# q and k multiplied by the decays channel by channel, and brought to heads through DRAM instead of by transposes

## The reference

```
mag = sqrt(a_re^2 + a_im^2);  a = (a_re, a_im) * min(mag, 0.999) / (mag + 1e-6)
for t in tokens:   S = a[t] * S + k[t] (x) v[t]        # complex S, 48 x 48 per head; k, v real
                   y[t] = q[t] . real(S)
```

## Time and profile before

| | |
|---|---|
| runs | 2439.87 us median of 3 (2435.78 to 2443.03) |
| profiled execution | 2443.79 us, its span 2442.0 us |
| TensorE busy | 2307.7 us, 95% of the span; granted clock 0.985 in the mean |
| VectorE, ScalarE, POOL busy | 1035.7, 763.4, 332.4 us |
| DMA | 106.63 MB in 95411 packets, 44 GB/s |

### The profile page before, as it was taken

One profiled execution on the slowest core, in us unless ns is written; L12 is line 12 of the kernel. 1 busy time (PEld: TensorE's weight loads), 2 busy tenths in 40 slices (PEclk: granted clock), 3 DMA queues, 4 the chain that ended last, 5 costly groups with the idle time before them and its releaser, 6 DMA issues.

```text
span 2442.0 us, 36281 instructions
## 1 busy us (share of the span) xinstructions
PE 2307.7 (95%) x14011; PEld 2150.2 (88%) x14011; DVE 1035.7 (42%) x2073; ACT 763.4 (31%) x1519; POOL 332.4 (14%) x423
## 2 busy tenths in 40 slices
PE   3699999999999899999999999999999999999999
PEld 3699999999999888998999999999999899989998
DVE  7787888888873333222222222222222222222222
ACT  3455555555545411222211222211222221222211
POOL 0000000000001211111111111111211111111100
PEclk8699999999999999999999999999999999999999
DMA  3211111111111400111011111041111110111001
GB/s 103 78 40 35 47 47 47 47 46 47 47 40 45 152 27 27 35 36 35 29 30 29 35 35 35 28 145 31 35 35 36 29 30 29 35 35 35 29 13 26
DMA packets 95411, 106.63 MB, mean 44 GB/s; under 512 B 9448, under 2 KB 89576, under 8 KB 95208
## 3 DMA queue, kind: packets, MB, share of 16 engines
q1 hardware_dynamic: 95208, 103.99, 13.8%
HBM read 89.80 MB, written 14.16 MB: 43 GB/s over the span
## 4 chain that ended last, share of the span: by engine, by line
PE 82%; DVE 8%; ACT 6%; issue 2%; DMA 1%; POOL 0%; SPq 0%; ACTq 0%; DVEq 0%
PE bank L1105 14%; PE bank L1106 14%; PE bank L1107 14%; PE bank L1224 11%; PE bank L1225 11%; PE bank L1226 11%; PE bank L1092 2%; PE bank L1091 2%; PE bank L1096 1%; PE bank L1086 1%; ACT ubuf L564 1%; ACT ubuf L566 1%; ACT ubuf L562 1%; PE bank L1081 1%; DVE an L707 1%
## 5 line engine op out<-in xcount | busy, mean ns | idle before, releaser
L660 ACT ACTIVATE h_h<-bank 128x512 fp32r<-128x512 f32 x384 | 229.8, 598 | 1254.7 <-PE bank L1107 1245.5
L1224 PE MATMUL bank<-w_h,h_h 128*128 128x384 f32 x1536 | 516.4, 336 | 0.0
L1226 PE MATMUL bank<-w_h,h_l 128*128 128x384 f32 x1536 | 516.3, 336 | 0.0
L1225 PE MATMUL bank<-w_l,h_h 128*128 128x384 f32 x1536 | 516.2, 336 | 0.0
L961 DVE SCALAR_TENSOR_TENSOR h_l<-bank,h_h 128x512 fp32r<-128x512 f32 x384 | 265.3, 691 | 530.2 <-ACT h_h L660 529.8
L490 POOL TENSOR_TENSOR w_l<-stage,w_h 128x256 fp32r<-128x256 f32 x384 | 286.2, 747 | 1296.4 <-ACT w_h L642 1296.2
L1105 PE MATMUL bank<-x2h,w_h 128*128 128x512 f32 x1152 | 451.1, 392 | 3.2 <-issue 2.4
L1106 PE MATMUL bank<-x2l,w_h 128*128 128x512 f32 x1152 | 451.1, 392 | 0.0
L1107 PE MATMUL bank<-x2h,w_l 128*128 128x512 f32 x1152 | 448.4, 389 | 0.0
L974 DVE SCALAR_TENSOR_TENSOR acc<-bank,prob,acc 128x384 f32<-128x384 f32 x168 | 103.8, 618 | 578.9 <-PE bank L1226 578.9
L1224 PEld LDWEIGHTS bank<-w_h,h_h 128*128 128x128 f32 x1536 | 288.1, 188 | 1.9
(11 more groups left out here) (134 smaller groups left out, 2771.5 us busy)
## 6 DMA issues: line engine op xcount, KB each, us to landing
stage<-w_ SPq DMA_DIRECT2D x384, 128.0 KB, 2.1
qb<-q_in_ SPq DMA_DIRECT2D x24, 192.0 KB
kb<-k_in_ SPq DMA_DIRECT2D x24, 192.0 KB
vb<-v_in_ SPq DMA_DIRECT2D x24, 192.0 KB
x_hi<-x2h_s SPq DMA_DIRECT2D x36, 128.0 KB, 1.9
x_lo<-x2l_s SPq DMA_DIRECT2D x36, 128.0 KB, 1.8
x2h<-x_hi SPq DMA_DIRECT2D x6, 768.0 KB, 8.7
x2l<-x_lo SPq DMA_DIRECT2D x6, 768.0 KB, 10.2
```

The source lines that it names most:

```text
L660: act.activation(h_h[:, f], hc[f % 3][:], ACT.Relu).then_inc(hh_done, 1)
L1224: pe.matmul(dst, h_h[:, f, t_], w2s[slot][0][:, f], start=f == 0, stop=False)
L1225: pe.matmul(dst, h_h[:, f, t_], w2s[slot][1][:, f], start=False, stop=False)
L1226: mm = pe.matmul(dst, h_l[:, f, t_], w2s[slot][0][:, f], start=False, stop=f == NF2 - 1)
```

## The change

**Products.** q and k themselves are transposed to channels (`q_turn`, `k_turn`, three transposes each), and VectorE multiplies them there: q by both parts of p in one instruction (`by_q`, into `qp`), k first by `rr` (into `pm`) and then by both parts of p (`by_k`, into `kp`). POOL's `pinv` is gone.

**To heads.** SP stores `qp` and `kp` to DRAM as [part, channel, token] and loads them back as `qs` and `ks`, with the 48 channels of a head on partitions 0 to 47 (real) and 48 to 95 (imaginary): two stores and four loads a unit, in pieces of 512 bytes. k with tokens on partitions (`kt`, for the state) comes from `ks` by eight transposes (`k_back`), copied by ScalarE (`k_by_token`).

**Order.** A unit has 9 steps on TensorE. Unit `u` carries the four tiles from `t = 4 * (u - 2) - 1`, and nine tiles follow behind unit 23. On TensorE three `mm_in` and two `mm_out` stand between the turns and `k_back`. The lists of ScalarE and VectorE are written anew. The gate goes to `att[2]`. `araw` and `r_sum` have more room, y a buffer of its own.

```diff
 def to_heads(u):                                   # SP, new
+    if u:
+        sp.wait_ge(qs_in, 32 * u)
+        sp.wait_ge(ks_in, 32 * u)
+    sp.wait_ge(dve_ev, u * DVE_EV + 1)
+    sp.dma_start(qk_d[0].rearrange("r (k p) t -> p r k t", k=KT), qp[:]).then_inc(q_stored, 16)
+    sp.wait_ge(kp_done, u + 1)
+    sp.dma_start(qk_d[1].rearrange("r (k p) t -> p r k t", k=KT), kp[:]).then_inc(k_stored, 16)
+    if u:
+        sp.wait_ge(step_done, (u - 1) * STEPS + 7)
+    sp.wait_ge(q_stored, 16 * (u + 1))
+    for r in range(2):
+        sp.dma_start(qs[r * D:(r + 1) * D], qk_d[0][r].rearrange("(h d) t -> d h t", h=H)).then_inc(qs_in, 16)
+    sp.wait_ge(k_stored, 16 * (u + 1))
+    for r in range(2):
+        sp.dma_start(ks[r * D:(r + 1) * D], qk_d[1][r].rearrange("(h d) t -> d h t", h=H)).then_inc(ks_in, 16)
...
 for u in range(UNITS):                             # SP
+    if u + 3 < UNITS:
+        load_a(u + 3)
     load_q(u + 1); load_k(u + 1)
-    if u % 2 == 0 and u + 3 < UNITS:
-        load_a(u + 3)
-    check_y(u)
-    if u % 2 == 0 and u >= 4:
-        store_x2(u // 2 - 2)
+    to_heads(u)
+    if u % 2 and u >= 5:
+        store_x2(u // 2 - 2)
+    check_y(u)
     load_v(u + 1)
-    if u % 2 == 0 and u + 4 < UNITS:
-        load_a(u + 4)
...
 def unit(u):                                       # ScalarE, new; t = 4 * (u - 2) - 1, ahead = u + 3 < UNITS
+    g_hi(t - 1); g_sq(t)
+    if even: p_sq(u + 1)
+    elif ahead: scale_sq(u + 3)
+    g_hi(t); g_sq(t + 1)
+    if even:
+        p_root(u + 1)
+        if ahead: scale_sq(u + 3)
+    elif ahead: scale_root(u + 3)
+    g_hi(t + 1); g_sq(t + 2)
+    k_by_token(u)
+    if not even: p_sq(u + 1)
+    y_out(u)
+    if even and u >= 4: x2_hi(u // 2 - 2)
+    g_hi(t + 2)
+    if even and ahead: scale_root(u + 3)
+    if not even: p_root(u + 1)
+    g_sq(t + 3)
+    x_hi(u)
...
 def by_q(u):                                       # VectorE, new; waits left out
+    dve.tensor_tensor(qp, att[0][:, 0:DM] (to both parts), p, ALU.mult).then_inc(dve_ev, 1)
 def by_k(u):
+    dve.tensor_tensor(flat, att[1][:, 0:DM], rr, ALU.mult).then_inc(dve_ev, 1)
+    dve.tensor_reduce(r_sum[0:1, u:u + 1], att[1][0:1, DM:DM + KT + 1], AX.X, ALU.add).then_inc(bound_done, 1)
+    dve.tensor_tensor(kp, flat (to both parts), p, ALU.mult).then_inc(kp_done, 1)
...
 def unit(u):                                       # VectorE, new; scans = odd and u + 1 < UNITS
+    by_q(u); by_k(u)
+    g_lo(t - 1)
+    if even: final(u + 1)
+    if scans: blocks(pair, 1, 4)
+    g_max(t)
+    if scans: blocks(pair, 4, 6)
+    if even: p_sum(u + 1)
+    g_lo(t)
+    if not even and u >= 5: gate_out(u // 2 - 2)
+    if even and u + 2 < UNITS: scale(u + 2)
+    if scans: blocks(pair, 6, NI); scan_init(pair); scan(pair, 0, 2)
+    g_max(t + 1)
+    if even: p_inv(u + 1)
+    if ahead: scale_sum(u + 3)
+    if scans: scan(pair, 2, 4)
+    g_lo(t + 1); g_max(t + 2)
+    if scans: final(u + 1)
+    masked(u)
+    if scans: p_sum(u + 1)
+    g_lo(t + 2)
+    if even and u >= 4: x2_lo(u // 2 - 2)
+    state_add(u)
+    if even and ahead: scale(u + 3)
+    if scans: p_inv(u + 1)
+    g_max(t + 3)
+    x_lo(u)
...
 for u in range(UNITS):                             # TensorE, new
+    q_turn(u); k_turn(u)
+    tile_in(t); tile_out(t); tile_in(t + 1)        # tile_out(t) is mm_out(t - 2)
+    if u % 2 and u >= 5:
+        pe.wait_ge(dve_ev, u * DVE_EV)
+        gate(u // 2 - 2)
+    tile_out(t + 1); tile_in(t + 2)
+    k_back(u, 0)                                   # waits for ks_in; the first half of k, into att[2]
+    k_back(u, 1)                                   # into att[0]
+    scores(u, 0)                                   # waits for qs_in; into att[1]
+    scores(u, 1)                                   # waits for k_by_token's first copy; into att[2]
+    tile_out(t + 2)
+    y_sum(u); state_sum(u)
+    tile_in(t + 3)
+    y_turn(u)
+    tile_out(t + 3)
```

More of the change, by code:

```diff
@@ L879, in unit @@
                 if scans:
-                    blocks(pair, 1, 5)
-                by_qk(u, 1)
-                if moe:
-                    g_lo(t)
+                    blocks(pair, 1, 4)
+                if t >= 0:
+                    g_max(t)
+                if scans:
+                    blocks(pair, 4, 6)
+                if even:
+                    p_sum(u + 1)
+                if t >= 0:
+                    g_lo(t)
+                if not even and u >= 5:
+                    gate_out(u // 2 - 2)
+                if even and u + 2 < UNITS:
+                    scale(u + 2)
+                if scans:
+                    blocks(pair, 6, NI)
+                    scan_init(pair)
+                    scan(pair, 0, 2)
+                if t >= -1:
                     g_max(t + 1)
                 if even:
-                    p_sum(u + 1)
-                    if u + 2 < UNITS:
-                        scale(u + 2)
+                    p_inv(u + 1)
+                    if ahead:
+                        scale_sum(u + 3)
                 if scans:
-                    blocks(pair, 5, NI)
-                    scan_init(pair)
-                    scan(pair, 0, 1)
-                if even and u >= 4:
-                    x2_lo(u // 2 - 2)
+                    if ahead:
+                        scale_sum(u + 3)
+                    scan(pair, 2, 4)
+                if t >= -1:
+                    g_lo(t + 1)
+                    g_max(t + 2)
+                if scans:
+                    final(u + 1)
                 masked(u)
@@ L897, in unit @@
                     first_lo(6 * u, 6 * u + 3)
-                if moe:
-                    g_lo(t + 1)
-                    g_max(t + 2)
-                if even:
-                    p_inv(u + 1)
-                    if u + 3 < UNITS:
-                        scale_sum(u + 3)
-                if scans:
-                    scan(pair, 1, 4)
-                state_add(u)
-                if moe:
-                    g_lo(t + 2)
-                if scans:
-                    final(u + 1)
-                if moe:
-                    g_max(t + 3)
                 if scans:
                     p_sum(u + 1)
+                if t >= -1:
+                    g_lo(t + 2)
+                if even and u >= 4:
+                    x2_lo(u // 2 - 2)
+                state_add(u)
+                if even and ahead:
+                    scale(u + 3)
+                if scans:
+                    p_inv(u + 1)
+                if t >= -1:
+                    g_max(t + 3)
                 if u < 3:
@@ L918, in unit @@
                 x_lo(u)
-                if even and u + 3 < UNITS:
-                    scale(u + 3)
-                if scans:
-                    if u + 3 < UNITS:
-                        scale_sum(u + 3)
-                    p_inv(u + 1)
             dve.wait_ge(filled, FILLS)
@@ new lines, in y_sum @@
+            def y_sum(u):
+                b = u % B
+                pe.wait_ge(act_ev, u * ACT_EV + 2)
+                pe.wait_ge(dve_ev, u * DVE_EV + 4)
+                pe.wait_ge(v_in, 16 * (u + 1))
+                for h in range(H):
+                    hd = slice(h * D, h * D + PAD)
+                    pe.matmul(att[0][:, hd], at[:, h], vb[:, hd], start=True, stop=False)
+                    mm = pe.matmul(att[0][:, hd], qs[0:96, h], state[0:96, b, hd], start=False, stop=True)
+                mm.then_inc(step_done, 1)
@@ new lines, in state_sum, with y_turn @@
+            def state_sum(u):
+                for h in range(H):
+                    hd = slice(h * D, h * D + PAD)
+                    mm = pe.matmul(att[1][0:96, hd], kt[:, h].rearrange("p r d -> p (r d)"), vb[:, hd],
+                                   start=True, stop=True)
+                mm.then_inc(step_done, 1)
+            def y_turn(u):
+                pe.wait_ge(act_ev, u * ACT_EV + 3)
+                pe.wait_ge(y_checked, u + 1)
+                turn(att[2], y).then_inc(step_done, 1)
```

344 lines of the change are left out of this document (157 added, 187 removed).

## The result

The changed kernel takes 2509.36 us (median of 4 runs, 2505.99 to 2512.1), the kernel before 2439.39 in the same session: a ratio of 1.0281, with a 95% interval from 1.0263 to 1.0299. It is slower by 2.8%; 2504 was predicted. The profiled execution takes 2510.08 us, its span is 2508.3, and TensorE's mean granted clock is 0.961, where it was 0.985. In what follows a stand is a time in which an engine waits with nothing to do.

The account below looks back on a forecast made before the run. TensorE was taken to set the pace, VectorE's new order to make it wait. Head +4, nine pairs +38, clock +14, units 21 to 23 +4, tail +4: +64 on 2443.8, 2508, as runs' median 2504; range 2435 to 2560.

Parts of the forecast that it names:

- The sum: Whole kernel: head +4, nine pairs +38, their clock +14, units 21 to 23 +4, tail +4; together +64 us.
- The walk: Units 3 to 20: both queues followed through one pair give 65.5 us against 61.3, +4.2 a pair.
- y in odd units released by `masked`: Expected sign in odd units: y starts when VectorE's `masked` ends, at 27.2 us behind `q_turn`.
- The clock: TensorE's stands in units 3 to 20 bring the low clock: +1.5 us a pair, between 0 and 5; +14 in all.
- the even unit's 2.8 us sometimes: Even units: TensorE's stand of 2.8 us brings the low clock only sometimes, within the +1.5 us a pair.
- The DRAM trip: From kp to `k_back`: 3.5 us each way, 8 with the issues, bounds 5 and 13; costs nothing in steady state.
- no wait of TensorE for `qs_in` or `ks_in` past unit 2: Expected sign: after unit 2 TensorE never waits for the loads of `qs` and `ks`.
- The head: Units 0 to 2: +3 for the open trip, +5 in unit 1, 4.3 less in unit 2; +4 us, -2 to +12.
- C: Rival, chance 0.03: the trip through DRAM holds the scores in the units; about 2590 us.
- E: Rival, chance 0.05: the walk counts some 5 us a pair too much, the pair stays near 61; 2445 us.
- D: Rival, chance 0.08: the clock is still low when y starts in odd units; +50 us, 2554.
- B: Rival, chance 0.12: TensorE stays the bound, pair of 54 us, about 2382; needs odd units' `masked` to end by 18.

Follow-up runs that it names:

- e1: The changed kernel with ScalarE's `k_by_token` moved ahead of `scale_sq` or `scale_root`, `g_hi` and `g_sq`: 2545.1 us, 1.0426 of the kernel before.
- e2: The changed kernel with VectorE's `masked` moved ahead of the last scan steps, `g_lo`, `g_max` and `final`: 2511.4 us, 1.0286 of the kernel before.
- e6: The changed kernel with unneeded matmuls (48 in odd, 16 in even units) between `scores(0)` and `scores(1)`: 2511.8 us, 1.0288 of the kernel before.
- e5: The changed kernel with `qs` and `ks` loaded from an input tensor at the unit's start, stores kept: 2502.4 us, 1.0255 of the kernel before.
- e8: e3's kernel with `qs` and `ks` loaded from an input tensor at the unit's start, stores kept: 2392.6 us, 0.9801 of the kernel before.
- after: The changed kernel itself, with the whole change and no further edit, against the kernel before: 2509.4 us, ratio 1.0281.
- e4: The kernel before with only VectorE's odd-unit list changed, three scan steps and `final` ahead of `masked`: 2547.6 us, 1.0434 of the kernel before.
- e3: The changed kernel with both `k_by_token` and `masked` moved forward, nothing else: 2400.9 us, 0.9839 of the kernel before.
- e9: e4's kernel with 44 matmuls that do nothing useful ahead of y in odd units: 2510.5 us, 1.0290 of the kernel before.

## Why the prediction was right, point by point

**The sum.** By VectorE's `by_q` of each unit the 66.3 us between the spans fall so: up to unit 3 +2.8 (predicted +4), nine pairs +57.0 (predicted 38 + 14 = 52), units 21 and 22 -0.6 and all behind them, unit 23 and the tail, +7.0 (predicted +4 for units 21 to 23 and +4 for the tail). Sum 66 against 64.

**The walk** was right almost to the tenth in the one pair whose even unit kept its clock, and for its reasons; the mean of the nine pairs is 67.8 us. `q_turn` to `q_turn` is 28.7 us even (predicted 28.9) and 36.8 odd (predicted 36.8) in the pair at 447.6, 65.56 together. The stand at `scores(1)` is 6.11 (6.2) and 2.05 (2.8; `k_back` had waited 0.9 for `ks` just before), for the copy predicted. `scale_sum` is done at 17.7 behind `q_turn` (17.9), `masked` at 26.9 (27.2), y starts at 27.4 (27.2). The operation with 768 elements takes 0.95 where 0.9 was taken, and `scale_sum` 0.55 everywhere.

**"y in odd units released by `masked`"** did not hold. `masked` ended at 503.25, and y began at 503.70 behind `mm_out` at the low clock; in the other odd units from 5 to 19 the distance is 0.8 us. That y came within 0.6 us of the 27.2 predicted is in part luck: the low clock stood in for `masked`. e1 and e2 show that neither can be taken away alone.

**The clock** is the term that was too small: +1.5 a pair was taken; 57.0 less nine times 4.1 (65.56 against 61.45 by the same marks) leaves 20 us, 2.2 a pair; e6's first half gives 2.5. The words "the even unit's 2.8 us sometimes" were the error. By `by_q` even units lasted 30.7 us where they kept the clock (that at 448.4) and 32.3 to 33.2 in the eight other pairs, 1.7 a pair in the mean. In odd units the low clock was mostly hidden, as predicted: 0.3 us in the one at 479.1 (34.9 against 34.6 in e6's first half), and 0.5 more in the others. The Trainium skill, "TensorE: Matmul & The Clock Gate", section "HAM oscillation — how this bites in real kernels", describes a matmul kernel whose wait between bursts is long enough that every round starts at the slow clock. The trace agrees for the stands of 6.1 us. That stands as short as 2.1 us bring it down too, in eight of nine even units, is shown by this trace and not by the page.

**The DRAM trip** was hidden, as the walk had it, though longer: 4.1 us for a store and 3.7 for a load against 3.5 each, and 9.2 from the end of kp (450.83) to `k_back` (460.03) against 8. So "no wait of TensorE for `qs_in` or `ks_in` past unit 2" was wrong in a small thing: `k_back` waited 0.9 us in even units. That costs nothing while `scores(1)` stands 2 us behind it; e5 and e8 bound the whole at 7 and 8 us.

**The head.** The first tile came at 106.46 (105.5 predicted, 97.59 before). y of unit 0 began 4.2 us later than before (55.10 against 50.93), 3 predicted for the open trip, and the other 4.7 come in unit 1, 5 predicted. There VectorE's list reached `masked` at 89.92 without a wait, and only the second half of it waited 0.5 us for the scores.

**Rivals.** C is excluded by e5, E by the length of the pair. D was not the case in after, whose y ran at full speed in steady state, but its mechanism is real: e1, e4 and the second half of e6 show y at the low clock, and 2545 in e1 is near D's 2554. B named its own point of decision, a `masked` that ends by 18 in odd units; in e3 it ends at 18.9, the pair is 56.5 us on average against B's 54, and the time 2401 against B's 2382. The change could be faster than before, by B's mechanism; two places in two lists decided that it was not.

What stays open: what decides that a stand of 1.7 to 2.4 us brings the clock down in one unit and not in the same place of another (after's even units, e6 before and from unit 13, the wait for the logits before and in e9).

## What to carry to other kernels

When an order written by hand changes, walk each engine's list to the operation that releases the pacing engine; that gave a pair to 0.1 us where the clock stayed up in its even unit, while counting the instructions saved gave the wrong sign. When a wait has been found, ask what holds the same piece next: two independent holds that end within a microsecond hide each other, and each edit alone gains nothing or loses. And look where a stand lies, not only how long it is: the same low clock costs well under 1 us in front of work that must wait anyway, and 3.5 to 5 us where it falls on the work that sets the pace.

## What was not expected of the hardware

- A stand of 2.1 us was enough to bring TensorE's clock down in eight of nine even units (0.62 in the window at 531.6); in that from 448 to 479 it was not.
- The clock fell late in a stand and came back only in the work behind it: 1.00 in the first window of the 6.11 us stand, 0.63, 0.50, 0.74 and then 1.00.
- Matmuls for nothing made two kernels faster by 37 and 51 us, and left a third where it was.
- The low clock behind a wait of 2.4 us that had been harmless in the kernel before made VectorE later in e9, though nothing there had been changed.
- Foreseen, and it came: `scale_sum`, 2.19 us beside POOL's `pinv`, takes 0.55 in all 24 units without it.
